# Attention scores per head on 64 rows each, one key-maximum instruction for two heads, and means sent earlier at the start

## The chip, the cores and the metric

The kernel runs on one core of a Trainium2 chip. The metric is device time in microseconds (us) of one launch. Three runs of the kernel before took 610.35, 611.28 and 612.75 us; their median is 611.28 us.

## The reference, cut to what matters

Inputs: q, k, v of shape (2, 8, 768, 64) in fp32, and weights of two mixing blocks. The attention of each of the 16 heads uses a window of 15 keys to either side plus 24 block summaries (of 32 keys each):

```
k_sum = k.reshape(B, H, nb, 32, D).max(axis=3)
v_sum = v.reshape(B, H, nb, 32, D).mean(axis=3)
scores_l = scale * q @ k^T, outside |i - j| < 16 set to -1e9
scores_s = scale * q @ k_sum^T + log(32)
a = softmax(concat[scores_l, scores_s])        # 1e-9 is added to the sum
x = a @ concat[v, v_sum]
```

x, put together to (2, 768, 512), then goes through a token mix (x + two matmuls over the tokens), a channel block of width 1536 with a residual, and a layer norm with a channel block of width 2048 and a residual. All of it is computed by the kernel in fp32, the channel blocks as three products of split fp32r parts.

## The kernel before, in words

The work of the attention is cut into 8 *pairs* (2 batches x 4 pairs of heads; the two heads lie on partitions 0 to 63 and 64 to 127) and each pair into 6 *tiles* of 128 queries, 48 tiles in all. The order of the work on each engine is written out by hand in one Python loop per engine, with semaphores between engines; nothing is scheduled by a program.

For a tile n the steps are:

- `scores(n)` on PE: one matmul of 128 rows (both heads) by 2 x 182 columns. A key row holds 158 window keys and 24 maxima; the keys lie block-diagonally in `k_sb` (each head has its own half of the columns, and the other half of its rows is zero, cleared once at the start by `clear_keys`). The result of both heads lands in one PSUM bank, `score_bank[n % 3]`, so three tiles can be under way.
- `mask_scores(n)` on DVE: per head one masked, scaled copy out of the bank with its row minimum.
- `exps(n)` on ACT: per head one exponential.
- `turn(n)` on PE: three transposes through the identity. `copy_turned(n)` on ACT takes them out of PSUM.
- `weigh(n)` on PE: one matmul with `v_far` (the 30 window edge rows and the 24 means of both heads, 108 rows) and two with `v_own`.
- after every third tile `normalise` on DVE divides by the sums.

PE's loop is scores(n + 3), turn(n + 1), weigh(n). DVE's loop is mask_scores(n + 3), then, where due, `normalise` (every third tile), `key_maxima` (tiles 0 and 1 of a pair, for the next pair, one head each), `tok_low_part` (tile 4 of the first four pairs: the low part of a token weight, which waits for `tok_high_part` on ACT, which in turn is queued there behind exps(n + 3)). From tile 25 on, matmuls of the first batch's token mix are put in behind `weigh`.

The maxima: DVE's `key_maxima` writes 24 maxima of a head into tile 0's columns of `k_sb`, and POOL's `spread_keys` copies them to the columns of the other five tiles (`k_ready`); scores of a new pair wait for it. The means: POOL's `sum_values` adds the 32 rows of each block in a tree of five instructions, PE turns the sums (`turn_sums`), ACT scales them (`copy_means`), and SP's queue sends them by two DMAs with 6-fold repetition into `v_far` (`send_means`). `weigh` of a pair's first tile waits for them.

At the start, SP's queue loads k, q and the turned v of pair 0; then v, once DVE has written the ones into `v_far` (from `v_init`, `far_init`); PE keeps busy with 16 bf16 matmuls on `warm`.

Names: a *bank* is 2 KB of PSUM per partition; `qk_done` counts score matmuls, `scored` the masked heads.

Of the kernel before, what the change touches and what calls it, by code (L numbers as in the profile page):

```python
# [22 lines left out]
NK = WIN + NSUM  # L23
PAIRS = H // 2
# [23 lines left out]
SUM_AT = (WIN, 0)  # L48
WIN_AT = (0, NSUM)
# [3 lines left out]
CLEARS = 2 * KB  # L53
WARM = 16
# [11 lines left out]
def build(nc, q_t, k_w, v_w, v_edge, v_t, w_tok1, w_tok2, w_ch1, w_ch2, w2_ch1, w2_ch2, gain, mask,  # L66
          value_init, identity, out):
    ctx = ExitStack()
    with ctx:
# [18 lines left out]
        with ExitStack() as a:  # L88
            mask_sb = sb(a, "mask_sb", [P, 3, NSUM + NK])
            q_sb = sb(a, "q_sb", [P, KB, S])  # L90
            k_sb = sb(a, "k_sb", [P, KB, 2, NT, NK])
# [6 lines left out]
            v_init = sb(a, "v_init", [2 * NB, PV])  # L98
# [27 lines left out]
        ld_init = sem("ld_init")  # L126
        far_init = sem("far_init")
# [10 lines left out]
        k_clear = sem("k_clear")  # L138
# [42 lines left out]
        pool_passed = sem("pool_passed")  # L181
# [15 lines left out]
        def clear_keys(engine, h, i):  # L197
            engine.memset(k_sb[64 * h:64 * h + 64, i, 1 - h], 0.0).then_inc(k_clear, 1)

        def span(r):  # L200
            b, k = divmod(r, 2 * PAIRS)
            p, g = divmod(k, 2)
            return b, slice(GT * g, GT * g + GT), slice(NT * b + GT * g, NT * b + GT * g + GT), slice(p * P, p * P + P)

# [4 lines left out]
        def _(sp):  # L209
            def load_k(r):  # L210
                i = r % KB
                if r >= KB:
                    sp.wait_ge(qk_done, NT * (r - KB + 1))
                for h in range(2):
                    sp.dma_start(k_sb[64 * h:64 * h + 64, i, h],
                                 k_w[r // PAIRS, r % PAIRS, 64 * h:64 * h + 64]).then_inc(ld_k[i], 16)

            def load_q(r):
                i = r % KB
                if r >= KB:  # L220
                    sp.wait_ge(qk_done, NT * (r - KB + 1))
                sp.dma_start(q_sb[:, i, :], q_t[r // PAIRS, r % PAIRS]).then_inc(ld_q[i], 16)

# [6 lines left out]
            def load_v(r):  # L230
                i, b, p = r % 2, r // PAIRS, r % PAIRS
                if r >= 2:
                    sp.wait_ge(pv_done, NT * (r - 1))
                else:
                    sp.wait_ge(far_init, r + 1)
                sp.dma_start(v_own[:, i], v_w[b, p]).then_inc(ld_v[i], 16)
                for h in range(2):
                    sp.dma_start(v_far[EDGE_ROW[h]:EDGE_ROW[h] + TAIL, i, :, 1 + h * D:1 + (h + 1) * D],
                                 v_edge[b, p, h]).then_inc(ld_edge[i], 16)

            def send_means(r):
                i = r % 2
                sp.wait_ge(mean_copied, r + 1)
                if r >= 2:
                    sp.wait_ge(pv_done, NT * (r - 1))
                for h in range(2):
                    at = SUM_ROW[h]
                    sp.dma_start(v_far[at:at + NSUM, i, :, 1 + h * D:1 + (h + 1) * D],
                                 v_mean[:, i, h * D:(h + 1) * D].rearrange("p (t n) -> p t n", t=1)
                                 .broadcast_to([NSUM, NT, D])).then_inc(ld_mean[i], 16)  # L250
# [16 lines left out]
            load_turned(0)  # L267
# [4 lines left out]
            send_means(0)  # L272
# [3 lines left out]
            for r in range(NPAIR):  # L276
# [6 lines left out]
                if r + 1 < NPAIR:  # L283
                    send_means(r + 1)
# [21 lines left out]
        def _(pool):  # L306
            def spread_keys(r):
                i = r % KB
                for h in range(2):
                    at = SUM_AT[h]  # L310
                    ks = k_sb[64 * h:64 * h + 64, i, h]
                    pool.wait_ge(kmax_done, 2 * r + h + 1)
                    pool.sem_inc(pool_passed)
                    nc.gpsimd.tensor_copy(ks[:, 1:NT, at:at + NSUM],
                                          ks[:, 0:1, at:at + NSUM].broadcast_to([64, NT - 1, NSUM])
                                          ).then_inc(k_ready, 1)
                pool.wait_ge(k_ready, 2 * r + 2)

            def sum_values(r):
# [4 lines left out]
                for j, n in enumerate(TREE):  # L324
# [6 lines left out]
                    else:  # L331
                        op.then_inc(tree_step, 1)
                        pool.wait_ge(tree_step, 4 * r + j + 1)
# [13 lines left out]
            for i in range(KB):  # L347
                clear_keys(nc.gpsimd, 1, i)
            pool.wait_ge(init_done, 3)
            pool.wait_ge(k_clear, CLEARS)  # L350
            spread_keys(0)
            sum_values(0)
# [12 lines left out]
        def _(pe):  # L365
# [12 lines left out]
            def scores(n):  # L378
                r, t = divmod(n, NT)
                i = r % KB  # L380
                if t == 0:
                    pe.wait_ge(ld_q[i], 16 * (r // KB + 1))
                    pe.wait_ge(ld_k[i], 32 * (r // KB + 1))
# [83 lines left out]
            for _ in range(WARM):  # L467
                mm(mix_bank[:], warm[:, 0:P], warm[:], True, True)
            pe.wait_ge(k_clear, CLEARS)
# [107 lines left out]
        def _(act):  # L577
# [84 lines left out]
            act.dma_start(v_init[:], value_init).then_inc(ld_init, 16)  # L662
            act.dma_start(mask_sb[:], mask).then_inc(ld_mask, 16)
            act.dma_start(ident[:], identity).then_inc(ld_ident, 16)
            act.dma_start(gain_sb[:], gain).then_inc(ld_gain, 16)
            exps(0)
            exps(1)
            copy_means(0, mix_bank[0:NSUM, mean_at])
# [36 lines left out]
        def _(dve):  # L705
# [3 lines left out]
            def key_maxima(r, h):  # L709
                i, at, win = r % KB, SUM_AT[h], WIN_AT[h] + HALO  # L710
                dve.wait_ge(ld_k[i], 32 * (r // KB + 1))
                ks = k_sb[64 * h:64 * h + 64, i, h]
                nc.vector.tensor_reduce(ks[:, 0, at:at + NSUM].rearrange("p (t n) -> p t n", t=NT),  # L713
# [259 lines left out]
```

## Time and profile before

| | us |
|---|---|
| median of 3 runs | 611.28 |
| profiled execution, its own time | 612.84 |
| span of the profile (first to last instruction) | 611.1 |
| outside the span | 1.7 |
| PE busy | 594.0 |
| PE weight loads busy | 484.1 |
| DVE busy | 219.8 |
| ACT busy | 159.4 |
| POOL busy | 49.6 |

The profile is of one execution. PE is busy for 97% of the span. The attention with the token mix of the first batch ends at about 113 us of the span; the rest is the token mix of the second batch and the two channel blocks, which the change doesn't touch. A matmul in fp32 is recorded as two instructions with a weight load each, so 48 score matmuls show as 96. Matmuls are pipelined: the duration of one holds a part that overlaps with the next, so the cost of one is read from the distance between starts.

### The profile page before, as it was taken

The page shows a single profiled execution, that of the slowest core. Times are in us where ns is not written, and L with a number is a line of the kernel's source. Part 1 is how long each engine was busy: PE and PEld are TensorE (multiplying, and loading weights), DVE is VectorE, ACT ScalarE, POOL GpSimd, SP SyncE. Part 2 cuts the span into 40 slices and gives each one's busy share as a digit, 9 for nine tenths or more (in the row PEclk, how much of TensorE's full clock was granted, in tenths as well). Part 3 has the DMA queues.
Part 4 walks back from the last instruction along what each step waited for, and adds up shares of the span by engine and source line. Part 5 has one row for each costly group of instructions (what it writes and reads, how often), then busy time and mean ns, then how long its engine had stood idle before and what let it go on. Part 6 is the DMA issues. An engine that isn't in the chain of part 4 may idle for free.

```text
span 611.1 us, 7428 instructions
## 1 busy us (share of the span) xinstructions
PE 594.0 (97%) x2808; PEld 484.1 (79%) x2808; DVE 219.8 (36%) x537; ACT 159.4 (26%) x331; POOL 49.6 (8%) x91
## 2 busy tenths in 40 slices
PE   6899999999999999999999999999999999999997
PEld 2677888878888788878888788888788888788886
DVE  5387666466334311134533632112521113211112
ACT  3376664334323101113332310112111102101110
POOL 5356541000000000000000000000000000000000
PEclk9799999999999999999999999999999999999999
DMA  8877532014333000000223100000100000100001
GB/s 231 226 210 225 168 106 96 17 35 137 104 104 104 1 0 1 0 1 8 96 103 104 34 2 2 0 1 0 70 0 1 0 1 0 70 1 0 1 0 69
DMA packets 21305, 35.58 MB, mean 58 GB/s; under 512 B 7596, under 2 KB 7832, under 8 KB 21272
## 3 DMA queue, kind: packets, MB, share of 16 engines
q1 hardware_dynamic: 20720, 34.69, 18.5%
q10 hardware_dynamic: 552, 0.44, 0.3%
q8 instruction: 22, 0.36, 0.2%
q14 instruction: 11, 0.09, 0.0%
HBM read 31.39 MB, written 3.15 MB: 57 GB/s over the span
## 4 chain that ended last, share of the span: by engine, by line
PE 92%; DVE 3%; issue 2%; DMA 2%; ACT 1%; POOL 0%; SPq 0%; DVEq 0%; ACTq 0%; POOLq 0%
PE bank L367 88%; PE bank L516 1%; DMA k_sb<-k_w 1%; DVE neg_scores L725 1%; DMA v_far<-v_mean 1%; PE bank L400 1%; PE bank L402 1%; PE bank L401 1%; DVE k_sb L713 1%; ACT probs L594 0%; DVE natural L844 0%; POOL v_tree L328 0%; ACT tok_w L610 0%; DVE x_split L707 0%; DVE natural L738 0%
## 5 line engine op out<-in xcount | busy, mean ns | idle before, releaser
L820 DVE SCALAR_TENSOR_TENSOR hidden<-bank,hidden 128x512 fp32r<-128x512 f32 x84 | 58.1, 691 | 309.3 <-ACT hidden L644 309.3
L367 PE MATMUL bank<-slots_late,hidden 128*128 128x512 f32 x648 | 156.4, 391 | 0.0
L644 ACT ACTIVATE hidden<-bank 128x512 fp32r<-128x512 f32 x84 | 50.2, 598 | 353.7 <-PE bank L367 353.7
L367 PEld LDWEIGHTS bank<-slots_late,hidden 128*128 128x128 f32 x648 | 120.9, 188 | 24.7
L367 PE MATMUL bank<-in_t,slots_late 128*128 128x512 f32 x576 | 137.7, 389 | 1.1 <-issue 1.1
L367 PEld LDWEIGHTS bank<-in_t,slots_late 128*128 128x128 f32 x576 | 107.9, 188 | 24.5 <-issue 2.3
L367 PE MATMUL bank<-in_t,slots_early 128*128 128x512 f32 x288 | 69.5, 390 | 0.0
L367 PEld LDWEIGHTS bank<-in_t,slots_early 128*128 128x128 f32 x288 | 54.1, 188 | 11.7
L367 PE MATMUL bank<-slots_early,hidden 128*128 128x512 f32 x216 | 51.9, 389 | 0.0
L367 PEld LDWEIGHTS bank<-slots_early,hidden 128*128 128x128 f32 x216 | 40.5, 188 | 8.4
L367 PE MATMUL bank<-k_sb,q_sb 128*128 128x364 f32 x96 | 39.7, 499 | 4.2 <-DVE neg_max L725 2.5
L594 ACT ACTIVATE probs<-neg_scores,neg_max 128x182 f32<-128x182 f32 x96 | 37.5, 441 | 14.6 <-DVE neg_max L725 14.3
L725 DVE CUSTOM_DVE_ANT_0 neg_scores<-bank,mask_sb 128x182 f32<-128x182 f32 x96 | 29.2, 342 | 20.5 <-PE bank L367 19.3
L367 PE MATMUL bank<-in_t,slots_kept 128*128 128x512 f32 x144 | 35.2, 396 | 1.0 <-issue 1.0
L367 PE MATMUL bank<-slots_kept,hidden 128*128 128x512 f32 x144 | 35.6, 396 | 0.0
L367 PEld LDWEIGHTS bank<-in_t,slots_kept 128*128 128x128 f32 x144 | 26.8, 187 | 8.2 <-issue 1.8
L367 PEld LDWEIGHTS bank<-slots_kept,hidden 128*128 128x128 f32 x144 | 27.0, 188 | 6.4
L603 ACT COPY probs_t<-bank 128x384 f32<-128x384 f32 x48 | 22.7, 472 | 31.9 <-PE bank L402 31.9
L367 PE MATMUL bank<-v_own,probs_t 128*128 128x65 f32 x192 | 27.5, 267 | 0.0
L367 PEld LDWEIGHTS bank<-v_own,probs_t 128*128 128x128 f32 x192 | 26.1, 197 | 0.0
L367 PE MATMUL bank<-v_far,probs_t 108*128 108x130 f32 x96 | 19.3, 283 | 4.3 <-DMA v_far<-v_mean 4.3
L367 PEld LDWEIGHTS bank<-k_sb,q_sb 128*128 128x128 f32 x96 | 16.5, 196 | 7.0 <-issue 5.0
(72 smaller groups left out, 430.0 us busy)
## 6 DMA issues: line engine op xcount, KB each, us to landing
stage<-w_ch SPq DMA_DIRECT2D x56, 256.0 KB, 2.7
k_sb<-k_w SPq DMA_DIRECT2D x16, 273.0 KB, 4.2
v_own<-v_w SPq DMA_DIRECT2D x8, 390.0 KB, 3.1
q_sb<-q_t SPq DMA_DIRECT2D x8, 384.0 KB, 4.9
v_turned<-v_t SPq DMA_DIRECT2D x8, 384.0 KB, 3.7
out<-natural SPq DMA_DIRECT2D x12, 256.0 KB, 2.1
tok_stage<-w_tok SPq DMA_DIRECT2D x4, 384.0 KB, 4.0
v_far<-v_edge SPq DMA_DIRECT2D x16, 45.0 KB, 2.9
```

The lines of the kernel that those rows point to most:

```text
L367: return nc.tensor.matmul(dst, lhs, rhs, start=start, stop=stop, skip_group_check=True)
L400: nc.tensor.transpose(tb[:, 0:P], pr[:, 0:P], ident[:])
L401: nc.tensor.transpose(tb[0:2 * NB, P:2 * P], pr[:, P:P + 2 * NB], ident[:])
L402: nc.tensor.transpose(tb[:, 2 * P:3 * P], pr[:, P + 2 * NB:2 * NK], ident[:]).then_inc(turned, 1)
L516: last = nc.tensor.transpose(in_bank[c % 2][:, j * P:(j + 1) * P], to_turn[:, j, c * P:(c + 1) * P], ident[:])
L594: nc.scalar.activation(probs[:, n % 2, h * NK:(h + 1) * NK], neg_scores[:, n % 2, h, :], ACT.Exp, bias=neg_max[:, n % 2, h:h + 1], scale=- ...
L603: nc.scalar.copy(probs_t[:, n % 2, :], turn_bank[n % 2][:, 0:3 * P]).then_inc(turned_copied, 1)
L644: nc.scalar.activation(hidden[:, f % HID_RING, 0, :], ch1_bank[f % 2][:, 0:GN], ACT.Relu).then_inc(hid_high, 1)
L713: nc.vector.tensor_reduce(ks[:, 0, at:at + NSUM].rearrange("p (t n) -> p t n", t=NT), ks[:, :, win:win + P].rearrange("p t (n s) -> p t n ...
L725: nc.vector.tensor_tensor_reduce(neg_scores[:, n % 2, h, :], score_bank[n % 3][:, h * NK:(h + 1) * NK], mask_sb[:, kind, (1 - h) * NSUM:(1 ...
L820: nc.vector.scalar_tensor_tensor(out=hidden[:, f % HID_RING, 1, :], in0=ch1_bank[f % 2][:, 0:GN], scalar=0.0, in1=hidden[:, f % HID_RING, ...
```

## The change

Four parts:

1. *Scores.* `scores(n)` issues two matmuls, one per head, each over that head's 64 rows and 182 columns, each into a bank of its own. The three score banks now go round by head, not by tile: head h of tile n uses bank (2n + h) % 3 and waits until the head three places earlier has been masked. `k_sb` has one block of 206 columns for both heads (24 maxima at the left for head 1, 158 window keys, 24 maxima at the right for head 0), loaded by one DMA on 128 partitions; the zeros and their clearing are gone. `qk_done` counts heads.
2. *Maxima.* One DVE instruction on 128 partitions, at tile 0 of a pair, writes the maxima of both heads to `k_max`; POOL copies them from there to all six tiles.
3. *Means of pair 0.* The turned v of pair 0 is the first load of ACT's queue; DVE sums it in one instruction; PE turns the sums between 13 and 6 warming matmuls, ahead of the first scores; ACT's queue sends the means, behind a wait for the ones.
4. *Ones.* The ones in `v_far` come by DMA (`value_ones`, and within `v_edge`), so v of pairs 0 and 1 is loaded without a wait, and an edge row is one piece of 3,120 bytes in place of six of 256.

```diff
+KW = NK + NSUM
-SUM_AT = (WIN, 0)
-WIN_AT = (0, NSUM)
+SUM_AT = (NK, 0)
+KEYS_AT = (NSUM, 0)
-WARM = 16
+WARM = (13, 6)
...
-            k_sb = sb(a, "k_sb", [P, KB, 2, NT, NK])
+            k_sb = sb(a, "k_sb", [P, KB, NT, KW])
+            k_max = sb(a, "k_max", [P, 2, NSUM])
...
+        def send_means(queue, r):
+            i = r % 2
+            queue.wait_ge(mean_copied, r + 1)
+            if r >= 2:
+                queue.wait_ge(pv_done, NT * (r - 1))
+            else:
+                queue.wait_ge(ld_ones, 32)
...
-                if n >= 3:
-                    pe.wait_ge(scored, 2 * (n - 3) + 2)
-                mm(score_bank[n % 3][:, 0:2 * NK].rearrange("p (h k) -> p h k", h=2), q_sb[:, i, t * P:(t + 1) * P],
-                   k_sb[:, i, :, t, :], True, True).then_inc(qk_done, 1)
+                for h in range(2):
+                    if 2 * n + h >= 3:
+                        pe.wait_ge(scored, 2 * n + h - 2)
+                    half = slice(64 * h, 64 * h + 64)
+                    mm(score_bank[(2 * n + h) % 3][:, 0:NK], q_sb[half, i, t * P:(t + 1) * P],
+                       k_sb[half, i, t, KEYS_AT[h]:KEYS_AT[h] + NK], True, True).then_inc(qk_done, 1)
...
+            for _ in range(WARM[0]):
                 mm(mix_bank[:], warm[:, 0:P], warm[:], True, True)
-            pe.wait_ge(k_clear, CLEARS)
+            pe.wait_ge(ld_ident, 16)
+            pe.wait_ge(init_done, 3)
+            turn_sums(0, mix_bank[:, mean_at])
+            pe.wait_ge(mean_copied, 1)
+            for _ in range(WARM[1]):
+                mm(mix_bank[:], warm[:, 0:P], warm[:], True, True)
             scores(0)
             scores(1)
             scores(2)
-            pe.wait_ge(ld_ident, 16)
-            pe.wait_ge(init_done, 3)
-            turn_sums(0, mix_bank[:, mean_at])
...
+            def key_maxima(r):
+                i, own = r % KB, NSUM + HALO
+                dve.wait_ge(ld_k[i], 16 * (r // KB + 1))
+                if r >= 2:
+                    dve.wait_ge(k_ready, 2 * (r - 1))
+                nc.vector.tensor_reduce(k_max[:, r % 2, :].rearrange("p (t n) -> p t n", t=NT),
+                                        k_sb[:, i, :, own:own + P].rearrange("p t (n s) -> p t n s", s=BLOCK),
                                         AX_X, ALU.max).then_inc(kmax_done, 1)
...
-                if t in (0, 1) and r + 1 < NPAIR:
-                    key_maxima(r + 1, t)
+                if t == 0 and r + 1 < NPAIR:
+                    key_maxima(r + 1)
```

On PE, in the middle of a pair, the rows of one loop turn (weigh, then scores of a tile three ahead, then turn) were, with k_sb as the keys and q_sb as the queries:

```order
L367 MATMUL bank2<-v_own,probs_t 128x65 x2
L367 MATMUL bank6<-k_sb,q_sb 128x364 [waits scored]
L400 MATMUL bank5<-ident,probs 128x128 [waits turned_copied,exp_done]
L401 MATMUL bank5<-ident,probs 108x128
L402 MATMUL bank5<-ident,probs 128x128
L367 MATMUL bank2<-v_far,probs_t 128x130 [waits turned_copied]
```

The same place on PE now, where the 64-row score matmuls stand:

```order
L351 MATMUL bank2<-v_own,probs_t 128x65 x2
L351 MATMUL bank1<-k_sb,q_sb 128x182 [waits scored]
L351 MATMUL bank6<-k_sb,q_sb 128x182 [waits scored]
L386 MATMUL bank5<-ident,probs 128x128 [waits turned_copied,exp_done]
L387 MATMUL bank5<-ident,probs 108x128
L388 MATMUL bank5<-ident,probs 128x128
L351 MATMUL bank2<-v_far,probs_t 128x130 [waits turned_copied]
```

One matmul became two, each with its own wait for `scored`, into two of the three banks.

On ACT, the start of the program was (DMA rows are transfers that ACT's queue issues):

```order
L662 DMA v_init<-value_init 108x130
L663 DMA mask_sb<-mask 128x618
L664 DMA ident<-identity 128x128
L665 DMA gain_sb<-gain 128x4
L594 ACT_TABLE_LOAD
L594 ACTIVATE probs<-neg_scores,neg_max 128x182 [waits scored] x4
L587 ACTIVATE v_mean<-bank 24x128 [waits mean_done]
L603 COPY probs_t<-bank 128x384 [waits turned]
```

The start of ACT's program now:

```order
L650 DMA v_turned<-v_t 128x768
L651 DMA ident<-identity 128x128
L652 DMA mask_sb<-mask 128x618
L654 DMA v_far<-value_ones 48x780 x2
L655 DMA gain_sb<-gain 128x4
L575 ACT_TABLE_LOAD
L575 ACTIVATE v_mean<-bank 24x128 [waits mean_done]
L208 DMA v_far<-v_mean 24x6x64 [waits ld_ones,mean_copied]
L208 DMA v_far<-v_mean 24x6x64
L582 ACTIVATE probs<-neg_scores,neg_max 128x182 [waits scored] x4
```

The copy of the means and their two DMAs moved ahead of the first exponentials, and a 393 KB load and the ones moved ahead of the mask and the gain.

## Rows read from the trace of the kernel before

**Rows 1.** The page: engine totals; the score matmuls' group.
```profile
PE 594.0 (97%) x2808; PEld 484.1 (79%) x2808; DVE 219.8 (36%) x537; ACT 159.4 (26%) x331; POOL 49.6 (8%) x91
...
L367 PE MATMUL bank<-k_sb,q_sb 128*128 128x364 f32 x96 | 39.7, 499 | 4.2 <-DVE neg_max L725 2.5
```
**Rows 2.** PE's waits in 0 to 130 us: total us, times, longest.
```profile
PE bank L367 <- DMA v_far<-v_mean: 4.3, 1, 4.3
PE bank L367 <- DVE neg_max L725: 2.5, 3, 1.0
```
**Rows 3.** Engine table of stretches: two pairs, then the mixing tiles.
```profile
core 0: us, PE busy (x) PEld busy (x) DVE busy (x) ACT busy (x) POOL busy (x), PEclk, DMA share, GB/s
35.96:46.69 10.73, 9.97 (x68) 8.17 (x68) 7.87 (x34) 7.80 (x21) 6.08 (x12) 1.00 0.73 212
...
63.90:92.60 28.70, 28.70 (x176) 23.46 (x176) 18.81 (x74) 18.00 (x46) 14.53 (x25) 1.00 0.46 136
```
**Rows 4.** Timeline of PE, tiles 13 to 15: start, us, what.
```profile
37.59 0.83 PE L367 MATMUL bank<-k_sb,q_sb 128*128 128x364 f32 x2
38.26 0.27 PE L400 MATMUL bank<-ident,probs 128*128 128x128 f32 x1
...
38.81 0.56 PE L367 MATMUL bank<-v_own,probs_t 128*128 128x65 f32 x4
39.20 0.83 PE L367 MATMUL bank<-k_sb,q_sb 128*128 128x364 f32 x2
...
40.81 0.83 PE L367 MATMUL bank<-k_sb,q_sb 128*128 128x364 f32 x2
```
**Rows 5.** Instructions that read k_sb and v_own, 36 to 60 us: ns min/median/max.
```profile
L367 PE MATMUL bank<-k_sb,q_sb x28: 468/496/545, 36.0 to 59.4; 128*128 128x364 f32 x28
...
L367 PE MATMUL bank<-v_own,probs_t x52: 222/274/275, 37.2 to 58.9; 128*128 128x65 f32 x52
```
**Rows 6.** Timeline around the token weight of pair 2.
```profile
38.64 0.35 DVE L725 CUSTOM_DVE_ANT_0 neg_scores<-bank,mask_sb 128x182 f32<-128x182 f32 x1 [0.99 <-PE bank L367]
...
39.84 0.82 ACT L610 CAST tok_w<-tok_stage 128x768 fp32r<-128x768 f32 x1
...
40.70 0.96 DVE L707 TENSOR_TENSOR tok_w<-tok_stage,tok_w 128x768 fp32r<-128x768 f32 x1 [1.44 <-ACT tok_w L610]
...
41.57 0.34 DVE L725 CUSTOM_DVE_ANT_0 neg_scores<-bank,mask_sb 128x182 f32<-128x182 f32 x1
```
**Rows 7.** Timeline ahead of pair 2's first scores (35.96).
```profile
32.80 0.94 DVE L713 TENSOR_REDUCE k_sb<-k_sb 64x24 f32<-64x768 f32 x1
...
33.07 1.00 POOL L342 TENSOR_TENSOR x_split<-natural,x_split 128x384 fp32r<-128x384 f32 x1
...
34.30 0.95 DVE L713 TENSOR_REDUCE k_sb<-k_sb 64x24 f32<-64x768 f32 x1
...
35.41 0.28 POOL L314 COPY k_sb<-k_sb 64x120 f32<-64x120 f32 x1 [0.88 <-DVE k_sb L713]
...
35.96 0.85 PE L367 MATMUL bank<-k_sb,q_sb 128*128 128x364 f32 x2 [1.00 <-DVE neg_max L725]
```
**Rows 8.** Timeline of the start, all engines (SPq is SP's queue).
```profile
1.40 0.36 ACTq L663 DMA_DIRECT2D mask_sb<-mask  x1
...
12.83 1.78 SPq L248 DMA_DIRECT2D v_far<-v_mean  x2
...
18.09 0.77 PE L367 MATMUL bank<-v_far,probs_t 108*128 108x130 f32 x2 [4.32 <-DMA v_far<-v_mean]
...
24.00 0.27 PE L400 MATMUL bank<-ident,probs 128*128 128x128 f32 x1
```
**Rows 9.** Chain that ended last, the transfer of pair 0's means: start, us.
```profile
13.76 4.19 DMA v_far<-v_mean
```
**Rows 10.** Engine table of the start, one stretch (columns as in rows 3).
```profile
18.00:20.00 2.00, 1.91 (x7) 1.79 (x8) 0.00 (x0) 0.00 (x0) 0.00 (x0) 0.50 0.92 224
```
**Rows 11.** DMA issues in 0 to 20 us: KB, us from issue to landing.
```profile
mask_sb<-mask ACTq DMA_DIRECT2D x1, 309.0 KB, 4.0
```

More of the change, by code:

```diff
@@ L212, in load_k @@
                 if r >= KB:
[L213 to L216, printed above, removed]
+                    sp.wait_ge(qk_done, 2 * NT * (r - KB + 1))
+                sp.dma_start(k_sb[:, i], k_w[r // PAIRS, r % PAIRS]).then_inc(ld_k[i], 16)
             def load_q(r):
@@ L233, in load_v @@
                     sp.wait_ge(pv_done, NT * (r - 1))
-                else:
-                    sp.wait_ge(far_init, r + 1)
                 sp.dma_start(v_own[:, i], v_w[b, p]).then_inc(ld_v[i], 16)
                 for h in range(2):
-                    sp.dma_start(v_far[EDGE_ROW[h]:EDGE_ROW[h] + TAIL, i, :, 1 + h * D:1 + (h + 1) * D],
+                    sp.dma_start(v_far[EDGE_ROW[h]:EDGE_ROW[h] + TAIL, i],
                                  v_edge[b, p, h]).then_inc(ld_edge[i], 16)
[L241 to L250, printed above, removed]
             def load_tok(k):
@@ L271, in _ @@
             load_q(1)
-            send_means(0)
             load_v(1)
@@ L283, in _ @@
                 if r + 1 < NPAIR:
-                    send_means(r + 1)
+                    send_means(sp, r + 1)
                 if r + KB < NPAIR:
@@ L309, in spread_keys @@
                 for h in range(2):
[L310 to L316, printed above, removed]
+                    half, at = slice(64 * h, 64 * h + 64), SUM_AT[h]
+                    pool.wait_ge(kmax_done, r + 1)
+                    nc.gpsimd.tensor_copy(k_sb[half, i, :, at:at + NSUM],
+                                          k_max[half, r % 2, :].rearrange("p (t n) -> p t n", t=1)
+                                          .broadcast_to([64, NT, NSUM])).then_inc(k_ready, 1)
                 pool.wait_ge(k_ready, 2 * r + 2)
@@ L660, in group @@
                     inputs_high(G + 1, 1 if norm else 0)
-            act.dma_start(v_init[:], value_init).then_inc(ld_init, 16)
+            act.dma_start(v_turned[:, 0, :], v_t[0, 0]).then_inc(ld_vt[0], 16)
+            act.dma_start(ident[:], identity).then_inc(ld_ident, 16)
             act.dma_start(mask_sb[:], mask).then_inc(ld_mask, 16)
-            act.dma_start(ident[:], identity).then_inc(ld_ident, 16)
+            for i in range(2):
+                act.dma_start(v_far[TAIL:TAIL + 2 * NSUM, i], value_ones).then_inc(ld_ones, 16)
             act.dma_start(gain_sb[:], gain).then_inc(ld_gain, 16)
+            copy_means(0, mix_bank[0:NSUM, mean_at])
+            send_means(act, 0)
             exps(0)
             exps(1)
-            copy_means(0, mix_bank[0:NSUM, mean_at])
             for n in range(-1, NTILE):
@@ L848, in _ @@
             dve.sem_inc(w_split, STAGES)
-            for i in range(KB):
-                clear_keys(nc.vector, 0, i)
+            nc.vector.memset(v_sum[:], 0.0).then_inc(init_done, 1)
             for i in range(2):
                 nc.vector.memset(turn_bank[i][96:P, P:2 * P], 0.0).then_inc(init_done, 1)
-            nc.vector.memset(v_sum[:], 0.0).then_inc(init_done, 1)
-            dve.wait_ge(ld_init, 16)
-            for i in range(2):
-                nc.vector.tensor_copy(v_far[:, i], v_init[:].rearrange("p (t v) -> p t v", t=1)
-                                      .broadcast_to([2 * NB, NT, PV])).then_inc(far_init, 1)
-            for h in range(2):
-                key_maxima(0, h)
+            dve.wait_ge(ld_vt[0], 16)
+            dve.wait_ge(init_done, 1)
+            nc.vector.tensor_reduce(v_sum[:, 0, 0:NSUM], v_turned[:, 0, :].rearrange("p (n s) -> p n s", s=BLOCK),
+                                    AX_X, ALU.add).then_inc(vsum_done, 1)
+            key_maxima(0)
             dve.wait_ge(ld_mask, 16)
@@ L915, in constants @@
         mask[:, kind, NSUM:NSUM + WIN] = np.where(there, 0.0, MASKED / SCALE)
[L916 to L919 removed]
+    value_ones = np.zeros((2 * NSUM, NT, PV), np.float32)
+    value_ones[0:NSUM, :, 0] = 1.0
+    value_ones[NSUM:, :, PV - 1] = 1.0
+    return mask, value_ones, np.eye(P, dtype=np.float32)
 def kernel(q, k, v, moe_w_tok1, moe_w_tok2, moe_w_ch1, moe_w_ch2, moe2_g_ln, moe2_w_ch1, moe2_w_ch2):
@@ L925 @@
     from concourse.bass_utils import run_bass_kernel_spmd as _run
-    mask, value_init, identity = constants()
+    mask, value_ones, identity = constants()
     def turned(a):
@@ L942, in value_windows @@
         own = np.ones((B, PAIRS, P, NT, PV), a.dtype)
-        edge = np.zeros((B, PAIRS, 2, TAIL, NT, D), a.dtype)
+        edge = np.zeros((B, PAIRS, 2, TAIL, NT, PV), a.dtype)
+        for h in range(2):
+            edge[:, :, h, :, :, h * (PV - 1)] = 1.0
         for t in range(NT):
@@ L963 @@
         "gain": np.ascontiguousarray(np.asarray(moe2_g_ln).reshape(C, P).T),
-        "mask": mask, "value_init": value_init, "identity": identity,
+        "mask": mask, "value_ones": value_ones, "identity": identity,
     }
```

49 lines of the change are left out of this document (15 added, 34 removed).

## The prediction

> **What bounds the kernel now.** I read the page first: PE is busy for 594.0 us, 97% of the span [rows 1]. Only the attention stage, to about 113 us, is touched, so I asked for PE's waits in the first 130 us. There are two that matter: one of 4.3 us for the means of pair 0, and three of 2.5 us together put down to DVE [rows 2]. The table by stretches says the rest: a pair of six tiles takes 10.73 us in the early part with PE busy for 9.97 of it, and from tile 25 on PE is never idle [rows 3]. So outside the start and three pair boundaries PE's own work is the time, and what a score matmul costs on PE decides.
>
> A tile's period is the distance between two score matmuls, 39.20 - 37.59 = 1.61 us, and the scores take 38.26 - 37.59 = 0.67 us of it [rows 4]. A score instruction has 364 columns and lasts 468 ns at least, one of 65 columns 222 ns [rows 5]: 299 columns more cost 246 ns, 0.82 ns each, and the part that doesn't grow is 222 - 53 = 0.17 us, which overlaps with the next. So the two instructions stream for 2 x 0.30 = 0.60 us, and 0.07 us are turnover.
>
> **The scores.** The new form has four instructions of 182 columns for the two of 364, 4 x 0.15 = 0.60 us of streaming if nothing overlaps: the same columns. It can only gain if the two heads, on different rows and in different banks, run beside each other. They are issued as a0, b0 (head 0), a1, b1 (head 1), in order. b0 needs the rows of a0, b1 those of a1; only a1 can run beside b0. That leaves three of four in line, 0.45 us, with 0.07 of turnover 0.52 us. Four weight loads must also come one after the other; v_own's matmuls of 65 columns, which stream for 0.05 us, follow each other every 0.11 us (0.56 us for four, of which 0.22 is the last), which I take for the time of a load [rows 4, 5]. a1's load is the third, ready 0.22 us after a0 starts and not 0.15: another 0.06. I take 0.58 us, a saving of 0.09 per tile. Bounds: all of one head beside the other is 0.30 + 0.07 = 0.37 us; the other end is no overlap, and at each of the two changes between 128 and 64 rows per tile PE runs dry for the 0.17 us that normally overlap: 0.67 + 0.34 = 1.01 us. No row of before shows either. The value is nearer the first, since the streaming part is measured and the order of issue is known. 48 tiles have 96 rows [rows 1]; the first four lie before PE's wait for the means and cost nothing, so 44 x 0.09 = 4.0 us gained; bounds 13 gained and 15 lost.
>
> No row shows two matmuls at once. The Trainium skill (TensorE: Matmul & The Clock Gate, Part 3) says that matmuls whose rows lie in different groups start about 4 ns apart and overlap fully; by it alone the scores would be near the low bound. The Trainium skill also says (TensorEngine Tiling (Array Packing), Key Properties) that changing the tiling mode drains TensorE; this kernel would do that twice a tile, and by it the scores would cost about 0.9 us. No run here shows it yet; it speaks for the second rival below.
>
> **The banks: a new wait.** Three banks by head are one and a half tiles. Head 1 of tile n may start only when head 0 of tile n - 1 has been masked. Before, scores had three tiles of room. At tile 4 of pairs 0 to 3 DVE stands still: after the masking at 38.64 it waits for ACT's high part (39.84, 0.82 us), does the low part (40.70, 0.96 us) and masks the next head only at 41.57, free at 41.57 + 0.27 + 0.08 = 41.92 [rows 6]. That head is head 0 of tile 14, and the scores of tile 15 started at 40.81 [rows 4], a second before. Now their second half has to wait. With tiles of 1.52 us it would start at 37.59 + 2 x 1.52 + 0.29 = 40.92, and DVE's chain ends 0.09 earlier at 41.83: 0.9 us of wait, four times, 3.6 us lost. Queued behind it on PE are turn and weigh, so nothing fills it. Bounds 0.6 to 1.3 each. Two instructions of 0.95 us on DVE being one helps elsewhere but not here.
>
> **The maxima.** The three boundary waits (1.00, and 0.76 twice, from the total of 2.5) are put down to DVE's masking, but that masked tile 11, and the scores of tile 12 need only tile 9: they wait for POOL's second copy, 35.41 + 0.28 = 35.69, which follows the second key_maxima of 34.30 [rows 7]. With one instruction at 32.80 the maxima are there at 33.75. POOL is then the last: its x_split ends at 34.07, and two copies of 0.28 to 0.3 us with 0.1 to 0.2 between end at about 34.9, with the 0.27 us to the scores 35.15; PE would be there at 34.96. I leave 0.3 us of each wait. Gained: 2.5 - 0.9 = 1.6 us; bounds 0.5 and 2.5. The two waits together thus lose 3.6 - 1.6 = 2.0 us. The DVE memsets and the eight saved maxima are off PE's path and cost and gain nothing else.
>
> **The start.** weigh(0) began at 18.09, after the means' DMAs were issued at 12.83 and the last had flown for 4.19 us [rows 8, 9]. Now the means are computed by about 8 us, but send_means waits for the ones, the fifth load of ACT's queue. That queue had moved the mask and 56 KB ahead of it, 0.37 MB, by 1.40 + 4.0 = 5.4 us [rows 8, 11], from the first data at about 2: near 0.11 MB per us. Now 393 + 66 + 316 + 300 = 1.07 MB come before: about 2 + 9.8, less because the other queue's share falls off; I take 11 us. The gain, on which the first masking waits, comes right behind the ones, so the masking of pair 0 starts no earlier than that. ACT then issues two DMAs of 0.89 us each (1.78 for two), to 12.8, before its first exponential; the flight of 2.2 to 4.2 us ends it at 15 to 17. I take 16: 2.1 us gained. From 18 to 24 us the clock was 0.50, the 1.2 GHz level, after 4.3 us in which PE stood still [rows 8, 10]: from 18.09 to the transposes at 24.00 are 5.9 us for two tiles of 1.61 and a transpose of 0.11. That is 2.6 us of half clock. PE still stands for some 2 us now, with sparse work before, so I count half of it, 1.3. Against it, all loads of pairs 0 to 2 now queue at once: a pair's 10.73 us at 212 GB/s is 2.3 MB [rows 3], and pair 0's token weight and pair 1's means lie behind some 6 MB, which at 224 to 280 GB/s arrive at 24 to 28 us, just when PE wants them; I take 0.8 back. Start: 2.6 us gained; bounds 1 lost (the ones or the gain late) and 5 gained.
>
> **Sum.** -4.0 (scores) + 3.6 (new wait) - 1.6 (maxima) - 2.6 (start) = -4.6 us. From the profiled 612.84 us that is 608.2; that execution was 1.56 us over the median, so against the median 611.28 I forecast 606.7. The end of the attention is PE's own work and the later stages follow it, so the gain reaches the end.
>
> **Rivals.**
>
> *Changing rows costs.* Place: the two changes between 128 and 64 rows per tile, 88 after the first four tiles. Price 0.17 us each, PE dry for the part that usually overlaps. Scores then cost 0.58 + 0.34 = 0.92 us, 44 x 0.25 = 11.0 us more than before; the new waits shrink to about 0.5 each as PE itself is slower (2.0 us). Sum +11.0 + 2.0 - 1.6 - 2.6 = +8.8, 620 us. With no overlap either it is some 4 more. It turns the sign from where scores cost 0.67 + 2.2/44 = 0.72 us. For it: scores, turn and weigh alternate, so nothing amortises a change; and PE is never idle to hide it. Against: transposes, 108-row and 128-row matmuls alternate now without a visible gap [rows 4].
>
> *No overlap, no cost.* Scores stay at 0.67, perhaps 0.04 more for two more turnovers: 0 to +1.8; waits +2.0, start -2.6: -0.6 to +1.2, 611.5 us. The change then doesn't do what it says. For it: fp32 takes two instructions per matmul, and the second of a head is in the way of the other head.
>
> *Start gives nothing.* As forecast, but ACT's queue is slow, the clock falls again: -4.0 + 2.0 + 0.3 = -1.7, 609.6 us.
>
> *Full overlap.* Scores at 0.37: -13 + 3.6 plus about 1 of longer token waits - 1.6 - 2.6 = -12.6, 598.7 us; DVE's chains per pair limit it.
>
> **Chances.** Forecast 0.45 (603 to 609), changing rows costs 0.24 (612 to 624), no overlap 0.16 (609 to 613), start gives nothing 0.08 (608.5 to 611), full overlap 0.07. What this kernel's runs can tell apart is about 0.5%, 3.1 us, so faster is below 608.2 and slower above 614.3. Faster: 0.40 + 0.07 + 0.03 = 0.50; slower: 0.21 + 0.02 = 0.23; same: 0.27. Range 600.5 to 619; the likeliest case's own range is 603 to 609.
>
> **What would show it.** In the profile after: the distance from a pair's first score instruction to the transpose behind it (0.58, against 0.92 or 0.67), and whether the start of head 1's first instruction lies less than 0.15 us behind that of head 0's second. Four waits of PE of about 0.9 us at the second half of scores, ended by DVE's masking; boundary waits down to 0.3. weigh(0) at about 16, and the granted clock of 16 to 24 us. The forecast is wrong if the scores cost over 0.72 us, or if the token waits are absent.

## The result, and the profile after

The changed kernel takes 645.89 us (median of 4 runs, 645.20 to 646.07) against 612.01 us for the kernel before: a ratio of 1.055, 95% interval 1.0523 to 1.0576. It is 34 us slower, outside the range of the prediction. Where runs of one kernel below differ by whether the clock fell in them, they are given one by one with their mean clock; a ratio leaves out those that lie over 1.5% above the kernel's fastest.

The page of the kernel after: engine totals, granted clock in 40 slices of 16 us, and the score matmuls.

```profile
PE 627.8 (98%) x2907; PEld 508.5 (79%) x2907; DVE 210.6 (33%) x525; ACT 159.3 (25%) x331; POOL 44.0 (7%) x83
...
PEclk8555559999999999999999999999999999999999
...
L351 PE MATMUL bank<-k_sb,q_sb 64*128 64x182 f32 x192 | 39.0, 492 | 3.6 <-DVE neg_max L717 3.6
```

Against [rows 1], PE is busy for 34 us more, although apart from three more warming matmuls it has no more columns to stream. The clock says why: five slices at 0.5, 1.2 GHz. The table by stretches of the kernel after (columns as in [rows 3]) gives the ends of this time.

```profile
10.00:20.00 10.00, 4.26 (x17) 2.62 (x16) 3.37 (x17) 3.89 (x10) 3.15 (x7) 0.62 1.03 351
...
30.00:40.00 10.00, 10.00 (x47) 8.43 (x46) 4.88 (x21) 4.97 (x13) 2.65 (x4) 0.50 0.29 104
...
80.00:90.00 10.00, 10.00 (x46) 8.43 (x47) 4.30 (x20) 4.63 (x12) 3.19 (x7) 0.50 0.33 112
90.00:100.00 10.00, 10.00 (x50) 8.03 (x49) 4.01 (x20) 4.17 (x13) 4.66 (x9) 0.62 0.47 138
100.00:110.00 10.00, 10.00 (x70) 7.25 (x68) 5.47 (x23) 5.53 (x15) 3.25 (x5) 1.00 0.45 157
```

From 30 us on PE doesn't stand still at all, and yet it works at half clock until about 97.6 us (a mean of 0.62 in 90 to 100 us), one microsecond behind the first mixing matmuls at 96.53. The kernel before also fell at its start, and that fall ended by itself at 24 us [rows 8, 10]. PE's timeline after, a tile at each level:

```profile
43.44 0.98 PE L351 MATMUL bank<-k_sb,q_sb 64*128 64x182 f32 x4
44.35 0.47 PE L386 MATMUL bank<-ident,probs 128*128 128x128 f32 x1
...
46.36 0.98 PE L351 MATMUL bank<-k_sb,q_sb 64*128 64x182 f32 x4
...
96.53 1.47 PE L351 MATMUL bank<-x_split,tok_w 128*128 128x512 f32 x3
...
100.29 0.58 PE L351 MATMUL bank<-k_sb,q_sb 64*128 64x182 f32 x4
100.80 0.33 PE L386 MATMUL bank<-ident,probs 128*128 128x128 f32 x1
...
102.65 0.58 PE L351 MATMUL bank<-k_sb,q_sb 64*128 64x182 f32 x4
```

A tile takes 46.36 - 43.44 = 2.92 us at half clock, against the 1.61 of [rows 4]. Three marks split the difference of the two spans, 643.4 - 611.1 = 32.3 us: the first weigh, the first mixing matmul, and the first one of the second batch.

| mark | before | after | stretch before | stretch after | difference |
|---|---|---|---|---|---|
| weigh(0) | 18.09 | 21.10 | 18.1 | 21.1 | +3.0 |
| first mixing (tile 25) | 65.58 | 96.53 | 47.5 | 75.4 | +27.9 |
| second batch's mixing | 115.49 | 147.95 | 49.9 | 51.4 | +1.5 |
| end | 611.1 | 643.4 | 495.6 | 495.5 | -0.1 |

25 tiles of 1.31 us more are 32.8; the kernel before loses 2.6 of its own to the half clock and 2.5 to boundary waits, and what remains, 27.7, is close to the 27.9. The 1.5 us of the next stretch are small but real: at the full clock a tile with mixing matmuls takes 102.65 - 100.29 = 2.36 us, against 2.31 in the kernel before:

```profile
66.36 0.77 PE L367 MATMUL bank<-k_sb,q_sb 128*128 128x364 f32 x2
...
68.67 0.77 PE L367 MATMUL bank<-k_sb,q_sb 128*128 128x364 f32 x2
```

The start is the second loss. Two rows of PE's waits, then two of the chain that ended last, where the row at 13.11 is the flight of pair 0's means:

```profile
PE bank L351 <- DVE neg_max L717: 3.6, 1, 3.6
PE bank L351 <- DMA v_far<-v_mean: 3.2, 1, 3.2
```

```profile
2.83 8.75 DMA v_far<-value_ones
...
13.11 7.86 DMA v_far<-v_mean
```

The ones landed at 11.6, as forecast (11). But the means then flew for 7.9 us, against 4.19 in [rows 9].

### The profile page after: what moved, and what is told of

It reads as the page before. It is cut to its first block, busy times and chain, and to the rows that moved or that the text cites. A ratio compares the mean times of both kernels' runs of the same rounds, so it can differ in the third digit from the quotient of the medians.

```text
span 643.4 us, 7597 instructions
## 1 busy us (share of the span) xinstructions
PE 627.8 (98%) x2907; PEld 508.5 (79%) x2907; DVE 210.6 (33%) x525; ACT 159.3 (25%) x331; POOL 44.0 (7%) x83
## 4 chain that ended last, share of the span: by engine, by line
PE 95%; DMA 3%; DVE 1%; ACTq 1%; issue 0%; ACT 0%
PE bank L351 88%; PE bank L386 2%; DMA v_far<-value_ones 1%; PE bank L504 1%; DMA v_far<-v_mean 1%; PE bank L387 1%; PE bank L388 1%; DVE natural L836 0%; PE bank L360 0%; ACTq L208 0%; DVE x_split L698 0%; DVE natural L730 0%; ACT x_split L603 0%; PE bank L448 0%; DVE h_tok L747 0%
## 5 line engine op out<-in xcount | busy, mean ns | idle before, releaser
L351 PE MATMUL bank<-k_sb,q_sb 64*128 64x182 f32 x192 | 39.0, 492 | 3.6 <-DVE neg_max L717 3.6
L351 PE MATMUL bank<-v_own,probs_t 128*128 128x65 f32 x192 | 37.1, 332 | 0.0
L351 PEld LDWEIGHTS bank<-v_own,probs_t 128*128 128x128 f32 x192 | 37.0, 269 | 0.0
L351 PEld LDWEIGHTS bank<-k_sb,q_sb 64*128 64x128 f32 x192 | 20.7, 255 | 14.4 <-issue 7.1
L351 PE MATMUL bank<-v_far,probs_t 108*128 108x130 f32 x96 | 25.3, 357 | 3.2 <-DMA v_far<-v_mean 3.2
```

The source lines that it names most:

```text
L351: return nc.tensor.matmul(dst, lhs, rhs, start=start, stop=stop, skip_group_check=True)
```

## The experiments

Each ratio is against runs of the kernel before that were taken together with the experiment; their medians are 611.65 us (b_rows64, b_split128, b_rows64_inline, a_keepwarm), 611.16 (b_modeswitch, a_dense, b_keepwarm_max0, b_early) and 612.60 (the rest).

**b_rows64: the scores alone.** The kernel before with only its scores changed.

```diff
+for h in range(2):
+    if 2 * n + h >= 3:
+        pe.wait_ge(scored, 2 * n + h - 2)
+    half = slice(64 * h, 64 * h + 64)
+    mm(score_bank[(2 * n + h) % 3][:, 0:NK], q_sb[half, i, t * P:(t + 1) * P],
+       k_sb[half, i, h, t, :], True, True).then_inc(qk_done, 1)
```

> The kernel before with only its scores changed: per head one 64-row matmul of 182 columns into one of three banks by head (start, maxima and ones as before). Theory A (the loop with 64-row scores cannot bring the clock back to 2.4 GHz once it has fallen): the clock falls at about 17 us as before and then stays at 0.50 until the dense mixing matmuls at tile 25; attention about 29 us longer, 640 us. Theory B (the long stay is caused by the other start of the changed kernel): the clock is back at about 24 us and the time is within 4 us of before, 608 to 616.

Measured: 642.07 us, ratio 1.0496 (1.045 to 1.0541). Theory A. The stretch long after the start:

```profile
60.00:80.00 20.00, 20.00 (x92) 16.64 (x90) 9.15 (x38) 8.98 (x23) 7.62 (x13) 0.50 0.51 144
```

So the scores carry 30 of the 34 us; the other parts together add some 3.5.

**b_split128: two matmuls, 128 rows.** As b_rows64, but with all rows (`q_sb[:, i, ...]`, `k_sb[:, i, h, t, :]`, the block-diagonal zeros in use).

> The kernel before with its scores as two matmuls of 128 rows and 182 columns, one per head, into three banks by head; no change of rows and no overlap. Theory A (64 rows or what comes with them is the cause): clock back at about 24 us, time 611 to 618, the excess being the 0.9 us waits for the token weight. Theory C (more and shorter instructions, or the banks by head, are the cause): clock stays at 0.50 to tile 25, 640 us or more.

Measured: 613.23 us, ratio 1.0033 (1.0011 to 1.0056). Theory A; neither the number of instructions nor the banks by head keep the clock down. This run fell too, but later, at about 29 us, behind a wait of 1.7 us, and came back some 3 us on while the loop ran. All ten runs have mean clocks of 0.991 to 0.997, so by an estimate from these none was low for more than about 11 us. The token wait is there. The period is also that of before: b_split128's scores take 0.67 us in a tile of 1.62 (36.02, 36.69 and 37.64 in its timeline), so four instructions cost no more than two.

```profile
30.00:40.00 10.00, 9.79 (x68) 9.38 (x67) 5.84 (x22) 6.13 (x16) 6.04 (x11) 0.87 0.58 179
40.00:50.00 10.00, 9.59 (x77) 9.51 (x78) 7.17 (x34) 7.70 (x20) 6.15 (x11) 1.00 0.73 206
```

```profile
39.26 0.53 PE L367 MATMUL bank<-k_sb,q_sb 128*128 128x182 f32 x2
40.41 0.58 PE L367 MATMUL bank<-k_sb,q_sb 128*128 128x182 f32 x2 [0.63 <-DVE neg_max L727]
```

**b_rows64_inline: no overlap, by a wait.** b_rows64 with one more line for the second head: `pe.wait_ge(qk_done, 2 * n + 1)`.

> As the 64-row scores put into the kernel before, but the second head's matmul waits until the first head's is done, so that nothing overlaps and PE streams the same number of columns one after the other. Theory A1 (rows in use count: half the rows, half the activity): clock stays low, over 645 us. Theory A2 (the overlap, which takes PE's streaming time out of the tile, is the cause): the clock comes back at about 24 us; scores cost about 0.9 us at the full clock, about 44 x 0.25 = 11 us more than before, 622 us.

Measured: 683.66 us, ratio 1.1161 (1.111 to 1.1212); the clock stayed at 0.50 to the first mixing matmuls at 119.98 and for 12 us beyond. Scores took 65.39 - 63.39 = 2.0 us a tile. It fits theory A1, but the wait also makes PE stand still for 0.15 us in each tile of 4.0 us (busy 19.25 us of 20), so it doesn't tell rows from gaps. b_rows64_same below does it without a wait.

**a_keepwarm: no standing still at the start.** The changed kernel with 18 warming matmuls ahead of the fourth head's wait and 22 ahead of weigh(0).

> The changed kernel with 18 and 22 more bf16 warming matmuls on PE, in its two long waits of the start (for the first masking, and for the means of pair 0), so that PE does not stand still there. Theory S (a fall at the start is all: the loop holds the high clock once it has it): clock 1.00 up to tile 25, time 612 to 616. Theory L (the loop itself does not hold it): the clock falls within some us after the warming ends and stays at 0.50 until tile 25; 640 us or more.

Measured: 614.98 us, ratio 1.0059 (1.0035 to 1.0083). Of ten runs, seven at a clock of 0.999 or 1.00 take 614.6 to 615.3; the other three lie at 618.4, 625.2 and 633.5 (clocks 0.994, 0.981, 0.965). Theory S, with a limit: mostly the loop holds the high clock once it has it, not always. 31 us of the 34 are back. Its timeline shows what the 64-row scores cost at 2.4 GHz, and one token wait:

```profile
25.31 0.58 PE L351 MATMUL bank<-k_sb,q_sb 64*128 64x182 f32 x4
25.82 0.33 PE L389 MATMUL bank<-ident,probs 128*128 128x128 f32 x1
25.99 0.27 PE L390 MATMUL bank<-ident,probs 128*108 128x128 f32 x1
...
26.43 0.56 PE L351 MATMUL bank<-v_own,probs_t 128*128 128x65 f32 x4
26.92 0.58 PE L351 MATMUL bank<-k_sb,q_sb 64*128 64x182 f32 x4
...
31.20 0.57 PE L351 MATMUL bank<-k_sb,q_sb 64*128 64x182 f32 x2 [0.50 <-DVE neg_max L723]
```

The period is 26.92 - 25.31 = 1.61 us, to a hundredth the one of [rows 4]. The score part shrank from 0.67 to 0.51, so the heads do overlap; but the first transpose behind it now takes 0.17 in place of 0.11, and from v_own's first to the scores it is 0.49 (26.43 to 26.92) in place of 0.39 [rows 4]. The two changes of rows give back 0.16, exactly what the score part gained.

**b_modeswitch: the gaps without the rows.** The kernel before with a 64-row matmul of 16 columns ahead of each 128-row score.

```diff
+mm(score_bank[n % 3][:, 0:16], q_sb[0:64, i, t * P:(t + 1) * P], k_sb[0:64, i, 0, t, 0:16], True, True)
```

> The kernel before (128-row scores of 364 columns, one bank per tile) with one more matmul of 64 rows and 16 columns ahead of each score matmul, into the same bank, where the score then overwrites it. It adds the two changes of row mode per tile without taking a row or a column away from the scores. Theory G (the gaps at the changes keep the clock down): after its fall at about 17 us the clock stays at 0.50 to tile 25, 640 us or more. Theory R (fewer rows at work, and two heads in the time of one, keep it down): the clock is back within about 10 us of weigh(0); the time is before plus the cost of the extra matmul and two changes, 48 x 0.2 to 0.35 = 10 to 17 us, 621 to 629.

Measured: 635.75 us median of 628.69, 635.75 and 637.63; ratio 1.0381 (1.0318 to 1.0444). The median lies above theory R's estimate and below the other's, so the clock has to decide, and it came back in the loop, at 33 us:

```profile
29.23 1.58 PE L367 MATMUL bank<-k_sb,q_sb 128*128 128x364 f32 x2
...
32.56 1.36 PE L367 MATMUL bank<-k_sb,q_sb 64*128 64x16 f32 x4
...
34.79 1.20 PE L367 MATMUL bank<-k_sb,q_sb 64*128 64x16 f32 x4
...
36.87 1.20 PE L367 MATMUL bank<-k_sb,q_sb 64*128 64x16 f32 x4
```

So the gaps at the changes don't keep it down to tile 25: theory R in the main. They may delay the return: it came 13.7 us after weigh(0) (19.30), not within the 10 I expected, and 5.8 us after it in the kernel before. The tile costs 36.87 - 34.79 = 2.08 us, 0.47 more than before and more than the 0.35 I allowed, which is some 23 us over 48 tiles. The run of 628.69 us, at a mean clock of 0.995, lies only 17.5 above the kernel before; this profile doesn't explain that one.

**a_dense: one more matmul per tile.** The changed kernel with one bf16 matmul of 128 x 512 in each of tiles 0 to 24.

> The changed kernel with one bf16 matmul of 128 rows and 512 columns more per tile, for tiles 0 to 24, ahead of weigh. It costs 25 x 0.21 = 5 us at the full clock. Theory A (the loop has too little PE activity to bring the clock back): with this activity the clock is back within some tens of us, and although PE has more to do, the kernel ends earlier: 620 to 632 against 645.9. Rival (once down, the clock stays down for a fixed or external reason until the mixing matmuls): about 651.

Measured: 657.64, 645.68 and 657.29 us at clocks of 0.924, 0.944 and 0.924. The expectation of theory A failed in size: one such matmul did not bring the clock back in the profiled run (657.64), and cost 12 us. In the run of 645.68 the clock was low for less time: by an estimate from the mean clocks 72 us in place of 100, so there it fell later or came back before tile 25. That run has no trace.

```profile
80.00:100.00 20.00, 20.00 (x86) 15.95 (x85) 7.38 (x32) 7.68 (x20) 6.17 (x11) 0.50 0.40 125
```

That left the rival open, a stay for a reason outside the loop. a_dense4 below answers it.

**b_rows64_same: both matmuls on rows 0 to 63.** b_rows64 with `half = slice(0, 64)` and head 0's keys for both.

> As the 64-row scores put into the kernel before, but both matmuls of a tile use rows 0 to 63 (head 0's scores are computed twice, head 1's are left out). Nothing can overlap and nothing waits; columns, instructions and banks are those of the 128-row pair. Theory rows (half the rows at work keeps the clock down): clock 0.50 from the start's fall to tile 25; scores at 1.2 GHz near 1.4 us a tile, so 650 to 660 us. Theory overlap (only the two heads in the time of one do it): the clock comes back within about 10 us of weigh(0); 612 to 622 us.

Measured: 673.53 and 670.97 us, ratio 1.0977 (1.0937 to 1.1017). Nothing overlaps (65.38 + 1.51 to the transposes at 66.89), PE never waits in the loop, and the clock stays down:

```profile
61.65 1.58 PE L367 MATMUL bank<-k_sb,q_sb 64*128 64x182 f32 x4
...
65.38 1.58 PE L367 MATMUL bank<-k_sb,q_sb 64*128 64x182 f32 x4
66.89 0.47 PE L402 MATMUL bank<-ident,probs 128*128 128x128 f32 x1
```

```profile
60.00:80.00 20.00, 20.00 (x77) 17.26 (x76) 7.69 (x30) 7.82 (x20) 5.54 (x10) 0.50 0.37 109
...
100.00:120.00 20.00, 20.00 (x69) 15.90 (x69) 7.16 (x25) 6.20 (x17) 6.12 (x11) 0.50 0.39 109
120.00:140.00 20.00, 20.00 (x84) 15.34 (x83) 7.65 (x29) 6.55 (x17) 4.39 (x8) 0.66 0.22 63
```

The same columns, instructions and banks as b_split128, half the rows, and with them the two changes of rows per tile. Theory rows; the overlap isn't needed for the stay. The time is above the 650 to 660, mostly because the clock didn't come back at tile 25: the first mixing matmuls start at 107.90, and the clock rises only at about 134 us, five tiles later. Each of these takes 4.9 us in place of 2.65 at the full clock, some 11 us in all. So the mixing matmuls end the stay, but not always at once.

**a_dense4: four per tile, for six tiles.** The changed kernel with four bf16 matmuls of 128 x 512 in each of tiles 0 to 5 only.

> The changed kernel with four bf16 matmuls of 128 x 512 more per tile, in tiles 0 to 5 only. One per tile had not brought the clock back. Theory A (too little activity of PE in the loop; the mixing matmuls of tile 25 end it by adding some, and once up it stays up): the clock is back during these six tiles, by about 45 us, and stays at 1.00 afterwards; about 28 us of the changed kernel's loss come back at a cost of up to 8: 620 to 628. If the clock falls again right after tile 5, or never rises: 650 or more.

Measured: 620.64 us (619.97 to 621.18), ratio 1.0134 (1.0109 to 1.0158), 25 us less than the changed kernel, with 24 matmuls more.

```profile
20.00:25.00 5.00, 3.84 (x16) 3.01 (x17) 0.62 (x4) 0.32 (x1) 2.55 (x5) 0.50 0.16 58
25.00:30.00 5.00, 5.00 (x29) 3.58 (x27) 0.62 (x4) 2.15 (x7) 0.00 (x0) 0.76 0.26 49
30.00:35.00 5.00, 5.00 (x37) 3.67 (x38) 2.07 (x11) 2.67 (x7) 1.50 (x2) 1.00 0.47 176
```

The clock rose at about 27 us, in the second tile with the four, and stayed up through the 19 tiles that have none. That refutes a reason outside PE's own work. The matmuls added here multiply zeros (`warm` is cleared at the start), so zeros are enough to bring the clock up.

**b_rows64_keepwarm: the other start.** b_rows64 with 6 and 18 warming matmuls in PE's two waits of the start.

> The kernel before with 64-row scores by head in banks by head, and warming matmuls (6 and 18) in PE's two waits of the start. If 64-row scores at the full clock cost as much per tile as before (overlap gained 0.16, two changes of rows lost 0.15): 1.00 clock, tile period 1.61, 609.5 for the kernel before without its fall, + 1 to 3 us for the token waits = 611 to 613. If it can win at the full clock: under 608.

Measured: 638.52, 636.37 and 638.55 us at 0.949 to 0.954, and 613.63 us at 0.997. The last is 0.6 us above the expected 611 to 613. The profile is of the first, and shows where that one lost the clock: at 2.4 GHz PE waited 1.7 us for DVE at tile 9 (31.83), and 1 us later the clock was down; a tile behind it takes 39.95 - 37.03 = 2.92 us.

```profile
29.56 0.57 PE L367 MATMUL bank<-k_sb,q_sb 64*128 64x182 f32 x2
31.83 0.57 PE L367 MATMUL bank<-k_sb,q_sb 64*128 64x182 f32 x2 [1.71 <-DVE neg_max L734]
...
37.03 0.98 PE L367 MATMUL bank<-k_sb,q_sb 64*128 64x182 f32 x4
...
39.95 0.98 PE L367 MATMUL bank<-k_sb,q_sb 64*128 64x182 f32 x4
```

This wait is the new one by banks of a head, so in this run the two faults of the change work together. b_split128 had the same wait of 1.7 us at the same tile and fell behind it too; only its return differs.

**b_keepwarm_max0: the kernel before, mended.** 20 warming matmuls in the wait for the means, both maxima at tile 0.

> The kernel before with 20 warming matmuls in PE's wait for the means of pair 0, and both instructions of key maxima at tile 0 of a pair. If the fall at 17 us costs 2.6 us and the three boundary waits come from POOL's second copy being late: clock 1.00 all through, boundary waits 0.3 us or less, 611.65 - 2.6 - 1.6 = 607.5. If the boundary waits are DVE's masking as the profile says: 609.

Measured: 610.76 us against 611.16, ratio 0.9995 (0.9977 to 1.0013): no difference. The boundary waits shrank from 2.5 to 1.4 us. Against that weigh(0) came later, at 18.98 in place of 18.09: the 20 warming matmuls, started at 14.67 at the full clock, take 4.3 us. Nor was the clock at 1.00 all through, as expected: it was low from 10 to 13.4 us, behind a wait of 2.1 us ahead of the first scores. One of the waits that stayed:

```profile
33.40 0.85 PE L367 MATMUL bank<-k_sb,q_sb 128*128 128x364 f32 x2 [0.47 <-DVE neg_max L729]
```

**b_early: early means for the kernel before.** The turned v of pair 0 loaded by ACT's queue, one DVE sum, means sent by SP ahead of pair 1's loads, ones as before, both maxima at tile 0, and 31 warming matmuls in four places.

> The kernel before with early means (v of pair 0 turned, by ACT's queue, summed by one DVE instruction, turned ahead of the scores, sent by SP's queue before the loads of pair 1), ones still copied by DVE, both maxima at tile 0, and warming matmuls in the waits. If what spoiled the early means of the changed kernel is the queue (ones and 6 MB of loads ahead of the 73 KB of means): weigh(0) at 14 to 15.5 in place of 18.09 and no fall of the clock, 603 to 606. If the flight of the means takes 7 us whatever is ahead of it: weigh(0) at 17 or later, 607 to 609.

Measured: 610.36 us, ratio 1.0 (0.9976 to 1.0023). The means left 2.8 us earlier, at 10.00 in place of 12.83 [rows 8], and weigh(0) began at 18.04, as before. But it was not the means that it waited for: PE works without a gap from 10.03 to 18.04. Warming matmuls at half clock put the first scores at 12.56, and ten more came behind them, the last five from 16.96 up to weigh(0). PE's one wait for means in this run, 1.0 us, is for pair 1's, at 28.96. So the means had landed by 18.04, at most 6.4 us after they were issued; whether an earlier weigh(0) would gain, the question of the run, stays open.

```profile
10.00 1.68 SPq L248 DMA_DIRECT2D v_far<-v_mean  x2
...
12.56 2.21 PE L365 MATMUL bank<-k_sb,q_sb 128*128 128x364 f32 x6
...
16.96 1.24 PE L365 MATMUL bank<-warm 128*128 128x512 bf16 x5
18.04 0.39 PE L365 MATMUL bank<-v_far,probs_t 108*128 108x130 f32 x2
```

**a_hold: fewer loads beside the means.** The changed kernel with gain and ones ahead of the mask, SP held until ones and mask have landed, 10 + 10 warming matmuls.

> The changed kernel with the gain and the ones ahead of the mask in ACT's queue, SP's loads of pair 1 held back until ones and mask have landed, and 10 + 10 warming matmuls in PE's waits. If the late weigh(0) of the changed kernel (21.1 us) comes from the ones landing at 11.6 and from the loads that its means' transfer shares the DMA engines with: ones by 9.5, flight of the means down from 7.9 to about 4, weigh(0) at 15 to 17, and with the clock up 609 to 612. If the flight is long by itself: weigh(0) at 18.5 or later, 613 to 615.

Measured: 613.43 and 614.63 us at clocks of 1.00 and 0.997, 645.17 and 645.67 at 0.939 and 0.936. The ones landed at 9.9, and the flight was still 8.1 us; weigh(0) at 19.67. The queue's order bought 1.4 us; the long flight is not explained by what I held back. And the very same kernel falls or doesn't: 32 us between two runs. The profiled one didn't, although PE stood still for 2.8 us ahead of weigh(0).

```profile
11.42 8.11 DMA v_far<-v_mean
```

## Why the prediction was wrong, point by point

*The fall of the clock at the start: the step that failed.* I read 2.6 us of half clock off the kernel before and carried it over: "That is 2.6 us of half clock ... so I count half of it, 1.3." The size and its sign were a property of the loop that followed. With 128-row scores the loop brings PE back to 2.4 GHz (before, b_split128, b_modeswitch); with 64-row scores it doesn't in any traced run of the plain loop, with overlap or without (after, b_rows64, b_rows64_same), until denser work comes (tile 25 or some tiles later, a_dense4). It cost 27.9 us, and no bound or rival of mine held it. The Trainium skill (TensorE: Matmul & The Clock Gate, Part 1) says that sustained activity of PE releases the clock; here PE was busy without a gap from 30 us on and the clock stayed at the lower level to 97 us, so the measurement decides: being busy in the profile isn't enough.

*The scores.* Forecast 0.09 gained per tile, measured at the full clock 0.00 in a plain tile and 0.05 lost in a tile with mixing: 4.0 us mis-sized, and about 1 more. The score part itself was better than forecast (0.51, not 0.58). I had three of the four instructions in line; the starts show two pairs (see the last section). I priced the overlap in the value, and the two changes of rows only in the rival, at 0.34; what shows of them outside the score part is 0.16. The rival "changing rows costs" had the right place at half the price. The Trainium skill (TensorEngine Tiling (Array Packing), Key Properties) says that changing the tiling mode drains TensorE. The trace agrees in kind: the row of weight loads of the 64-row scores, in the kernel after, starts with the matmuls at 100.29, 0.36 us after the load before it, and not ahead of them:

```profile
100.29 0.30 PEld L351 LDWEIGHTS bank<-k_sb,q_sb 64*128 64x128 f32 x4 [0.36 <-issue]
```

*The new wait by banks.* Right in place and kind: a wait at the second half of scores, ended by DVE's masking, four times. Its size at the full clock is 0.50 three times and 0.82 once, not 0.9, 2.3 us in all and not 3.6 (a_keepwarm). With 128 rows one is 0.63 and the four are 3.7 in all, 1.7 of it at tile 9 (b_split128). At half clock it vanishes (after, b_rows64): a tile then takes 2.92 us, and DVE keeps up.

*The maxima.* With both heads' maxima in one instruction the boundary waits are gone altogether in a_keepwarm, 2.5 us against the forecast 1.6; the reason, POOL's second copy, fits. With two instructions at tile 0 (b_keepwarm_max0) 1.4 us of the three stay.

*The start.* The ones as forecast, the flight of the means not: 7.9 us against 2.2 to 4.2, and weigh(0) at 21.1 against 16, 3.0 lost in place of 2.1 gained. I took the flight from a row in which the means were in the same queue as the loads; there they took 2.2 to 4.2 us (before, b_rows64, b_modeswitch). In ACT's queue, which held nothing else by then (0.08 MB in 11 to 21 us, beside 3.41 MB of SP's), they took 7.7 to 8.1 us in four kernels (after, a_dense, a_dense4, a_hold). That small pieces of 256 bytes in turn with large ones of another queue are served slowly would fit, but is only argued; it stays open.

What else stays open: why it is the rows. b_rows64_same and b_split128 differ in the rows and in the two changes of rows that come with them, and b_modeswitch has the changes and came back. So the 64-row scores are shown as the cause of the stay in this loop, and the changes alone as not enough; that they add to it isn't excluded, since b_modeswitch came back late. What PE's clock control counts isn't shown. And whether a start falls, or a wait of 1.7 us or 2.8 us makes the clock fall, differs between runs of one kernel (a_hold).

No kernel tried here beats the one before. Its own runs at a mean clock of 1.00 lie between 609.5 and 610.9 us, those at 0.994 between 611.6 and 613.7, but for one of 610.6: for this kernel a fall of the clock at the start costs some 2 us.

## What to carry to other kernels

Before making PE's work lighter per unit of time, by fewer rows or by packing, look at where the granted clock falls and what brought it back: a fall that heals in 6 us in one loop can last for 75 us in a lighter one, and a few dense matmuls just after it are cheap insurance (24 of them bought 25 us here). Price a change of rows in the forecast itself, 0.10 us into the 64-row matmuls and 0.06 out of them here, since it took all that two heads at once had gained. And a transfer's flight time holds only for the queue and company in which it was seen.

## What the runs showed of the hardware that was not expected

- PE was busy for 100% of 67 us at a granted clock of 0.50 (after, 30 to 97 us). The clock was up within two tiles when four 128 x 512 bf16 matmuls per tile were added (a_dense4), but not in the traced run with one (a_dense).
- Two 64-row fp32 matmuls on different halves do run together. In a_keepwarm two of a tile's four instructions have begun by 25.34 and still two by 25.57, and four by 25.58, so they start in pairs 0.26 us apart, though each head's second follows its first in the program:

```profile
25.31 0.42 PE L351 MATMUL bank<-k_sb,q_sb 64*128 64x182 f32 x2
```

- The plainest proof of the overlap is b_rows64_same, the same instructions on the same half: 1.51 us at the lower clock against 0.91 (44.35 - 43.44) in the kernel after, and 0.81 (134.73 - 133.92) at the full clock against 0.51. One behind the other, 64-row scores are dearer than 128-row ones (0.81 against 0.67).
- 0.26 us for a pair is hardly less than twice the 0.15 us that 182 columns take by the slope of [rows 5]: the tile's scores shrank from 0.67 to 0.51 us, by a quarter and not by half.
- A 64-row matmul of only 16 columns, put ahead of a 128-row one, cost 0.47 us per tile (b_modeswitch).
